# Zeros for the experts' rows in four transfers, issued with the first expert's weights behind single local tiles of the attention

## The chip, the cores and the metric

The kernel runs on one core of a Trainium2 chip. The metric is device time in microseconds (us) of one execution. All times of the profile are us from the first instruction of the span, unless ns stands beside them.

## The reference, cut to what matters

Three layers follow one another. Everything is float32.

- Attention over q, k, v of shape (2, 8, 576, 64). One part pools q, k and v by 4 along the sequence (144 positions), attends over them and repeats each result row 4 times. The other part lets each query attend to the keys fewer than 4 positions away. Their sum, 1152 tokens of 512 values, is x.
- A layer of 8 experts with top-1 routing. `w_gate` (512 x 8) gives logits, each token goes to its best expert, which takes at most 288 tokens (`capacity`), in order of the token number. An expert computes `relu(x @ w1) @ w2`, with 1024 hidden values. The result is multiplied by the token's gate probability.

```
for i in range(N):
    e = expert_idx[i]
    if counts[e] < capacity:
        disp[e, counts[e]] = x[i]
        ...
h = np.maximum(np.einsum('ecd,edf->ecf', disp, w1), 0.0)
y = np.einsum('ecf,efd->ecd', h, w2)
```

- A feed-forward layer: `h = x @ w_in` (2048 wide), `g = h * tanh(softplus(h))`, `g @ w_out`.

## The kernel before, in words

The five engines and SyncE (which issues the plain DMAs) each run a program of their own; semaphores order them. Tokens are split into 9 tiles of 128.

**Attention, 0 to about 102 us.** The work is a list `STEPS` of 15 steps: 9 local tiles ("local", t) and 6 parts of the pooled attention ("down", ...), in the order local 0 to 3, three down, local 4, three down, local 5 to 8. A loop over 19 rounds runs on TensorE, ScalarE and VectorE. In round n, TensorE computes the scores of step n (`scores`), transposes the probabilities of step n - 1 (`probs_t`) and multiplies those of an older step with v (`attend`): a down step two rounds after its scores, a local tile t in round t + 8. So local tiles 0 to 4 wait for their attend until the pooled rows are there; their probabilities, transposed, are kept in the buffer `raw` (`kept_probs`): tile t in unit `min(t, 3)`, so that tiles 3 and 4 share unit 3. `raw` has four units of 1 MB, and each later takes a quarter of an expert's weights (w1 in units 0 and 1, w2 in units 2 and 3). A unit may be loaded once the attend of the tile that it holds is done. The semaphore `s_av` counts attends, and `RANK` gives each one's place in that count.

After its attend (TensorE), tile t is copied to `x_sb` (ScalarE, `x_copy`, L686), transposed (`x_transpose`, L1302), copied (`xT`), multiplied by `w_gate` (`logits`), and VectorE computes its expert, its place and its gate (`route`, `read_counts`, `place`), and multiplies the tile by the gate (L1016, semaphore `s_gx`).

**Rows by expert.** The gated rows go to a DRAM tensor `x_by_expert` (`xe_dram` in the code), 288 rows of 512 values for each expert, and behind them 1152 rows that take the rows of dropped tokens. GpSimd scatters tile after tile with an indirect DMA (L627), after it has placed the pooled rows for all down steps (`place_od`, L592). The 2304 rows of the experts must be zero where no token lands, so SyncE first writes zeros to all of them (L472). The source is tile 8 of `x_sb`, which GpSimd has set to zero (`s_xz`) and which nobody writes until the end of the attention. The scatters, and the copy of tile 8 into `x_sb` in round 16, wait for these zeros (`s_zf`). When six scatters have landed, SyncE reads the first 256 rows of expert 0 (`load_full(0)`), and TensorE transposes them (`early_rows`); tiles 6 to 8 are added to them from `x_sb` by a matrix product with a one-hot matrix (`late_rows`), without DRAM.

**SyncE's program** up to the experts is a plain list: q and k, the pooled v, `w_gate`, the windows of v (`vwin`, L448), slot numbers (L470), then the zeros and the four units of expert 0 (L472, L477), then `load_full(0)` and the rest. Each issue runs in that order; a wait holds up all that stands behind it.

**Experts, about 114 to 263 us.** A loop over 8 experts: 64 matmuls with w1, 64 with w2, while SyncE loads the next expert's units as they become free. **Feed-forward, to the end.** Three sweeps over 384 tokens each, every product in three matmuls of float32r halves.

Of the kernel before, what the change touches and what calls it, by code (L numbers as in the profile page):

```python
# [7 lines left out]
P = 128  # L8
# [13 lines left out]
DM = H * D  # L22
E, FE = 8, 1024
# [10 lines left out]
NT = N // P  # L34
# [78 lines left out]


EARLY = 6


LAG_X = 8
HELD = NT // 2
KEPT = HELD + 1  # L120
# [6 lines left out]
def local_step(t):  # L127
    return STEPS.index(("local", t))
# [9 lines left out]
RANK = {m: i for i, m in enumerate(ATT)}  # L138
# [6 lines left out]
def build(nc, q, k, v, w_gate, w1, w2, w_in, w_out, consts, consts16, slot_nos, out, cap):  # L145
    tok_dram = nc.dram_tensor("token_of_slot", (N, 1), U32, kind="Internal").ap()
    CAP = cap

    xe_dram = nc.dram_tensor("x_by_expert", (E * CAP + N, DM), F32, kind="Internal").ap()
# [9 lines left out]
    with ctx:  # L159
        def alloc(stack, name, shape, dt, **kw):  # L160
            return stack.enter_context(nc.sbuf_tensor(name, shape, dt, **kw))

        def sem(name):
            return ctx.enter_context(nc.semaphore(name))
# [41 lines left out]
        x_sb = alloc(att, "x_sb", [P, NT, DM], F32)  # L206
# [29 lines left out]
        wo_in = alloc(exp_mem, "wo_in", [P, 2, DM], F32)  # L236
        slot_oh = alloc(exp_mem, "slot_oh", [P, NT - EARLY, SLOTS], F32)
        exp_mem.close()
# [27 lines left out]
        s_pt, s_ptc, s_av, s_avc = sem("probsT"), sem("probsT_copied"), sem("attn_out"), sem("attn_out_copied")  # L266
# [4 lines left out]
        s_xz, s_zf, s_xg, s_xet = sem("x_tile_zeroed"), sem("x_rows_zeroed"), sem("expert_x_in"), sem("expert_x_transposed")  # L271
# [63 lines left out]
        def od_copies(n):  # L335

            _, b, c, hh = STEPS[n]
            first = 0 if b == 0 else NT // 2 + 1
            cols = slice(hh * 4 * D, (hh + 1) * 4 * D)
            if c == 0:  # L340
                return [(vwin[OD_ROWS:P, 2 * (first + u):2 * (first + u) + 2, cols], slice(32 * u, 32 * u + 32)) for u in range(3)]
            out_ = []
            for half in range(2):
                cols = slice(half * 4 * D, (half + 1) * 4 * D)
                out_.append((vwin[OD_ROWS:P, 2 * (first + 3):2 * (first + 3) + 2, cols], slice(BLK * half, BLK * half + 32)))
                out_.append((vwin[OD_ROWS:P, BPB - 1 + b:BPB + b, cols], slice(BLK * half + 32, BLK * half + 64)))
            return out_
# [25 lines left out]
        def expert_units(e):  # L373

            a = w1[e].rearrange("(k p) f -> p k f", p=P)
            b = w2[e].rearrange("(k p) d -> p k d", p=P)
            return [a[:, :, 0:FE // 2], a[:, :, FE // 2:FE], b[:, 0:M1 // 2, :], b[:, M1 // 2:M1, :]]
# [43 lines left out]
        def _(sp):  # L421
# [45 lines left out]
            for g in range(BPB, NB):  # L467
# [1 line left out]

            sp.dma_start(slot_no[:, :], slot_nos).then_inc(s_sno, 16)  # L470
            sp.wait_ge(s_xz, 1)
            sp.dma_start(xe_dram[0:E * CAP, :].rearrange("(p a) d -> p a d", p=P),  # L472
                         x_sb[:, NT - 1, :].unsqueeze(1).to_broadcast([P, E * CAP // P, DM])).then_inc(s_zf, 16)

            def load_unit(e, i):

                sp.dma_start(raw[:, i, :].rearrange("p (k f) -> p k f", k=K1), expert_units(e)[i]).then_inc(s_raw[i], 16)  # L477

            for i in range(4):
                sp.wait_ge(s_av, RANK[local_step(i if i < 3 else KEPT - 1)] + 1)  # L480
                load_unit(0, i)

            def load_full(e, landed):

                sp.dma_start(xg[:, 0:XT - 1, :], xe_dram[bass.ds(e * CAP, FULL), :].rearrange("(a p) d -> p a d", p=P)
                             ).then_inc(landed, 16)
# [17 lines left out]

            sp.wait_ge(s_scat, 16 * EARLY)
            load_full(0, s_xg0)
# [52 lines left out]
        def _(pool):  # L559
# [26 lines left out]
            def place_od(n):  # L586

                pool.wait_ge(s_avc, RANK[n] + 1)
                done = od_placed(n - 1)
                for dst, rows in od_copies(n):  # L590
                    src = od[rows, n % 2, :].unsqueeze(1).to_broadcast([32, dst.shape[1], 4 * D])
                    nc.gpsimd.tensor_copy(dst, src).then_inc(s_odv, 1)  # L592
                    done += 1
                    pool.wait_ge(s_odv, done)
# [22 lines left out]
            for n in range(NS):  # L617
                if is_down(n):
                    place_od(n)
            pool.wait_ge(s_zf, 16)  # L620
            for t in range(NT):
                pool.wait_ge(s_gx, t + 1)
                if t == EARLY:
                    pool.wait_ge(s_xg0, 16)
# [56 lines left out]
        def _(act):  # L681
# [3 lines left out]
            def copy(dst, src):  # L685
                return nc.scalar.activation(dst, src, ACT.Copy)  # L686
# [35 lines left out]
            def x_copy(m):  # L722
                t = STEPS[m][1]
                act.wait_ge(s_av, RANK[m] + 1)
                if t == NT - 1:
                    act.wait_ge(s_zf, 16)
                copy(x_sb[:, t, :], ps[:, XB, :]).then_inc(s_avc, 1)

            def xt_copy(t):
# [138 lines left out]
        def _(dve):  # L868
# [14 lines left out]
            def pooled(t):  # L883


                def red(dst, src):
                    return V.tensor_reduce(dst, src.rearrange("p h (s f) -> p h s f", f=FACTOR), X, ALU.add)  # L887
                dve.wait_ge(s_qTc, t + 1)
                dve.wait_ge(s_kTc, t + 1)
                turn = ((HELD + 1) * P - S) // FACTOR  # L890
                for _, b, r0, n in tok_pieces(t):
                    lo, s0, cnt = b * S + r0, r0 // FACTOR, n // FACTOR
                    qcol = s0 if b == 0 else SDP + (s0 - turn if s0 >= turn else SD + s0)
                    kcol = b * SD + s0
                    red(qdT[:, :, qcol:qcol + cnt], qT[:, :, lo:lo + n])
                    last = red(kdT[:, :, kcol:kcol + cnt], kT[:, :, HALO + lo:HALO + lo + n])
                last.then_inc(s_qd, 1)
# [63 lines left out]
            def need(count):  # L961
                dve.wait_ge(s_r, count)
# [31 lines left out]
            def place(t):  # L994
# [10 lines left out]
                need(row)  # L1005
                if t >= EARLY:
                    if t == EARLY:
                        dve.wait_ge(s_sno, 16)
                    V.tensor_scalar(slot_oh[:, t - EARLY, :], slot_no[:, :], -float(E * CAP), r_a[:, c], ALU.add, ALU.is_equal
                                    ).then_inc(s_xoh, 1)  # L1010
# [159 lines left out]
        def _(pe):  # L1170
# [36 lines left out]
            def scores(n):  # L1207
                s0 = 2 * (n % 2)
                if STEPS[n][0] == "down":
                    _, b, c, hh = STEPS[n]  # L1210
                    for j in range(2):
                        if j == 1:
                            between(n)
                        for par in range(2):
                            for rows, q0, half in ([(slice(0, QA), 0, hh)] if c == 0 else
                                                   [(slice(BLK * i, BLK * i + BLK), QA, i) for i in range(2)]):
                                hp = 2 * half + j
                                r = slice(D * par, D * par + D)
                                q_ = qdT[r, hp, b * SDP + q0:b * SDP + (QA if c == 0 else SDP)]
                                last = mm(ps[rows, s0 + par, j * SD:(j + 1) * SD], q_, kdT[r, hp, b * SD:(b + 1) * SD], True, True)  # L1220
                else:
                    t = STEPS[n][1]
                    var = {0: 1, NT // 2: 2, NT - 1: 3}.get(t, 0)
                    for par in range(2):
                        mm(ps[:, s0 + par, 0:4 * WIN].rearrange("p (h w) -> p h w", h=4), identb[:, :],
                           maskb[:, var, :].unsqueeze(1).to_broadcast([P, 4, WIN]), True, False)
                    for hp in range(HP):
                        if hp == HP // 2:
                            between(n)
                        for j in range(2):  # L1230
                            for par in range(2):
                                r = slice(D * par, D * par + D)
                                c0 = t * P + j * BLK
                                last = mm(ps[j * BLK:(j + 1) * BLK, s0 + par, hp * WIN:(hp + 1) * WIN],
                                          qT[r, hp, c0:c0 + BLK], kT[r, hp, c0:c0 + WIN], False, True)
                last.then_inc(s_sc, 1)
# [332 lines left out]
```

## Time and profile before

| | us |
|---|---|
| three runs | 471.12, 474.72, 475.45 |
| median | 474.72 |
| the profiled execution, time | 477.65 |
| its span, first to last instruction | 475.5 |

Mean granted clock of TensorE in the profiled execution is 0.968 of 2.4 GHz. Busy shares of the span: TensorE matmul 94%, weight load 87%, VectorE 59%, ScalarE 48%, GpSimd 29%. The chain that ended last lies 84% on TensorE. In the rows further down, "issue" ahead of an instruction is idle time in which the engine waited for nothing that the profile shows; "remote" is a wait whose releaser the profile can't name. PE is TensorE's matmuls, PEld its weight loads.

### The profile page before, as it was taken

The numbers are of one execution on the slowest core, as the hardware profiler recorded it, in microseconds if no ns is written. First come the engines' busy times: TensorE is split into PE (matmuls) and PEld (weight loads), VectorE is DVE, ScalarE is ACT, GpSimd is POOL, SyncE is SP. The second block draws the span as 40 slices with busy tenths as digits, with TensorE's granted clock in tenths as the row PEclk, the third lists the DMA queues.
The fourth block names the chain that finished last, engine by engine and source line by source line (L and its number), as shares of the span: only waits on it lengthen the run. The fifth ranks groups of instructions, "written<-read, shape, count | busy, mean of one in ns | idle before, by whom it ended". The sixth has DMA issues, their size and how long they took to land.

```text
span 475.5 us, 10038 instructions
## 1 busy us (share of the span) xinstructions
PE 447.9 (94%) x3380; PEld 412.8 (87%) x3381; DVE 280.7 (59%) x665; ACT 230.1 (48%) x631; POOL 137.2 (29%) x136
## 2 busy tenths in 40 slices
PE   8869898989879999999999999999999999999993
PEld 7658687878879999999999898899988999988982
DVE  7879577679202102102111599888888888888873
ACT  2756665642313323332223566655665655656541
POOL 9587325111000000000004455433253333433202
PEclk9979899599989999999999999999999999999998
DMA  9999999232867988996846234123141121321001
GB/s 186 196 193 152 166 379 347 101 112 74 293 240 243 357 300 281 350 311 207 281 159 207 82 88 45 43 88 90 44 143 57 49 83 45 90 110 44 1 0 66
DMA packets 72143, 74.97 MB, mean 158 GB/s; under 512 B 32816, under 2 KB 47920, under 8 KB 72112
## 3 DMA queue, kind: packets, MB, share of 16 engines
q1 hardware_dynamic: 70384, 69.84, 51.0%
q0 software_dynamic: 1728, 4.72, 2.6%
q8 instruction: 18, 0.29, 0.3%
q14 instruction: 13, 0.11, 0.1%
HBM read 65.11 MB, written 9.44 MB: 157 GB/s over the span
## 4 chain that ended last, share of the span: by engine, by line
PE 84%; DVE 6%; ACT 4%; issue 3%; DMA 1%; SPq 1%; POOLq 0%; POOL 0%; ACTq 0%; DVEq 0%
PE ps L1174 79%; ACT pr L703 2%; PE ps L1256 2%; PE ps L1421 1%; DMA qk_tok<-in_q 1%; PE ps L1302 1%; SPq L431 1%; DVE mx L928 1%; DVE sme L935 1%; PE ps L1251 0%; DVE qT L901 0%; ACT prT L686 0%; DVE kdT L887 0%; DVE qdT L887 0%; DVE gL L1080 0%
## 5 line engine op out<-in xcount | busy, mean ns | idle before, releaser
L637 POOL TENSOR_TENSOR wiL<-raw,wiH 128x512 fp32r<-128x512 f32 x48 | 62.5, 1303 | 251.5 <-ACT wiH L686 148.3
L1174 PE MATMUL ps<-xe,raw 128*128 128x128 f32 (+2 forms) x512 | 71.7, 302 | 4.7 <-issue 3.9
L1174 PEld LDWEIGHTS ps<-xe,raw 128*128 128x128 f32 x512 | 70.4, 194 | 5.6 <-issue 4.4
L1174 PE MATMUL ps<-hid,raw 128*128 128x128 f32 (+2 forms) x512 | 70.8, 297 | 0.0
L1174 PEld LDWEIGHTS ps<-hid,raw 128*128 128x128 f32 x512 | 69.0, 191 | 0.0
L1174 PE MATMUL ps<-x2H,wiH 128*128 128x384 f32 x192 | 65.1, 339 | 0.3 <-DVE x2L L1080 0.3
L1174 PE MATMUL ps<-x2L,wiH 128*128 128x384 f32 x192 | 65.3, 340 | 0.0
L1174 PE MATMUL ps<-x2H,wiL 128*128 128x384 f32 x192 | 64.6, 337 | 0.0
L1174 PE MATMUL ps<-woH,gH 128*128 (+1 forms) x144 | 56.9, 395 | 2.5 <-DVE gL L1080 2.5
L1174 PE MATMUL ps<-woH,gL 128*128 (+1 forms) x144 | 57.2, 397 | 0.0
L1174 PE MATMUL ps<-woL,gH 128*128 (+1 forms) x144 | 56.7, 394 | 0.0
L1080 DVE TENSOR_TENSOR woL<-wo_in,woH 128x1024 f32 x8 | 9.8, 1226 | 79.4 <-ACT woH L686 79.4
L825 ACT ACTIVATE md<-mg 128x384 f32<-128x384 f32 x48 | 25.3, 526 | 43.8 <-DVE mg L1139 43.7
L781 ACT ACTIVATE hid<-ps 128x128 f32<-128x128 f32 (+2 forms) x64 | 18.8, 301 | 56.2 <-PE ps L1174 53.8
L1117 DVE TENSOR_SCALAR mu<-ps 128x384 f32<-128x384 f32 x48 | 26.7, 557 | 25.4 <-PE ps L1174 24.2
L1174 PEld LDWEIGHTS ps<-x2H,wiH 128*128 128x128 f32 x192 | 36.0, 188 | 2.5 <-issue 0.5
L1174 PEld LDWEIGHTS ps<-x2L,wiH 128*128 128x128 f32 x192 | 36.1, 188 | 1.9
L1080 DVE TENSOR_TENSOR x2L<-ps,x2H 128x128 f32 (+2 forms) x32 | 9.1, 321 | 46.0 <-ACT x2H L686 46.0
L1174 PEld LDWEIGHTS ps<-x2H,wiL 128*128 128x128 f32 x192 | 36.0, 188 | 0.0
L686 ACT ACTIVATE gH<-ps 128x384 fp32r<-128x384 f32 x47 | 23.2, 493 | 24.3 <-DVE ps L1151 24.3
L703 ACT ACTIVATE pr<-ps,mx 128x70 f32<-128x70 f32 (+2 forms) x96 | 30.6, 343 | 8.3 <-DVE mx L928 5.2
L1174 PEld LDWEIGHTS ps<-woH,gH 128*128 128x128 f32 x144 | 27.0, 187 | 8.0 <-DVE gL L1080 3.7
(140 smaller groups left out, 769.1 us busy)
## 6 DMA issues: line engine op xcount, KB each, us to landing
raw<-in_moe_w SPq DMA_DIRECT2D x32, 1024.0 KB
raw<-in_moe_w_in SPq DMA_DIRECT2D x24, 512.0 KB
x_by_expert<-x_sb SPq DMA_DIRECT2D x1, 4608.0 KB, 15.5
xg<-x_by_expert SPq DMA_DIRECT2D x8, 512.0 KB, 3.6
wo_in<-in_moe_w_out SPq DMA_DIRECT2D x8, 512.0 KB
v<-in_v SPq DMA_DIRECT2D x4, 576.0 KB
qk_tok<-in_k SPq DMA_DIRECT2D x8, 256.0 KB, 4.8
qk_tok<-in_q SPq DMA_DIRECT2D x8, 256.0 KB, 5.1
```

The costliest lines, as they stand in the source:

```text
L431: d = sp.dma_start(qk_tok[p0:p0 + n, slot3, i, :].rearrange("p (h d) -> p h d", h=H), src[b, :, r0:r0 + n, :].rearrange("h s d -> s h d"))
L637: nc.gpsimd.tensor_tensor(wiL[:, r, :, :], raw_wi_tile(r), wiH[:, r, :, :].bitcast(F32), ALU.subtract).then_inc(s_wil, 1)
L686: return nc.scalar.activation(dst, src, ACT.Copy)
L703: last = nc.scalar.activation(pr[0:rows, n % 2, a, h * w:(h + 1) * w], ps[0:rows, 2 * (n % 2) + a, h * w:(h + 1) * w], ACT.Exp, bias=mx[0: ...
L781: nc.scalar.activation(hid[:, m, 0:w], ps[:, m % 4, 0:w], ACT.Relu).then_inc(s_hr, 1)
L825: nc.scalar.activation(d, mg[:, r1, :], ACT.Ln, bias=2.0).then_inc(s_ln, 1)
L928: V.tensor_reduce(st(mx), sc, X, ALU.max, negate=True).then_inc(s_mx, 1)
L935: V.tensor_scalar(st(sme), st(sm), f, f * EPS, ALU.mult, ALU.add).then_inc(s_den, 1)
L1080: V.tensor_tensor(dst, whole, high.bitcast(F32), ALU.subtract).then_inc(sem_, 1)
L1117: V.tensor_scalar(mu[:, r, :], ps[:, 3 + r, 0:SW], MISH_CAP, None, ALU.min).then_inc(s_uc, 1)
L1174: return T.matmul(out_, a, b, start=start, stop=stop, skip_group_check=True)
L1256: last = T.transpose(ps[0:WIN, 6 + h // 4, (h % 4) * P:(h % 4 + 1) * P], pr[:, n % 2, h % 2, (h // 2) * WIN:(h // 2 + 1) * WIN], ident)
```

## The change

Before, the zeros are one transfer of 4608 KB, issued at once when `x_sb`'s last tile is zero, and units 0, 1, 2, 3 are issued behind the attends of local tiles 0, 1, 2 and 4. Now the zeros are four transfers of 576 rows (1152 KB) each, read from 96 instead of 128 partitions, six rows from each. The first is issued where the single one was. Then SyncE waits for the attends of local tiles 1 to 6 in turn and issues: behind tile 1 unit 0; behind tile 2 zeros 1; behind tile 3 unit 1 and zeros 2; behind tile 4 zeros 3; behind tile 5 unit 2; behind tile 6 unit 3. Both waits for the zeros want all four transfers.

```
--- before.py
+++ after.py
@@ -113,6 +113,11 @@
 
 
 EARLY = 6
+
+
+ZERO_PARTS, ZERO_P = 4, 96
+UNIT_BEHIND = {1: 0, 3: 1, 5: 2, 6: 3}
+ZERO_BEHIND = {2: 1, 3: 2, 4: 3}
 
 
 LAG_X = 8
@@ -469,16 +474,26 @@
 
             sp.dma_start(slot_no[:, :], slot_nos).then_inc(s_sno, 16)
             sp.wait_ge(s_xz, 1)
-            sp.dma_start(xe_dram[0:E * CAP, :].rearrange("(p a) d -> p a d", p=P),
-                         x_sb[:, NT - 1, :].unsqueeze(1).to_broadcast([P, E * CAP // P, DM])).then_inc(s_zf, 16)
+
+            def zero_rows(i):
+
+                rows = E * CAP // ZERO_PARTS
+                per = rows // ZERO_P
+                sp.dma_start(xe_dram[i * rows:(i + 1) * rows, :].rearrange("(p a) d -> p a d", a=per),
+                             x_sb[0:ZERO_P, NT - 1, :].unsqueeze(1).to_broadcast([ZERO_P, per, DM])).then_inc(s_zf, 16)
+
+            zero_rows(0)
 
             def load_unit(e, i):
 
                 sp.dma_start(raw[:, i, :].rearrange("p (k f) -> p k f", k=K1), expert_units(e)[i]).then_inc(s_raw[i], 16)
 
-            for i in range(4):
-                sp.wait_ge(s_av, RANK[local_step(i if i < 3 else KEPT - 1)] + 1)
-                load_unit(0, i)
+            for t in range(1, 7):
+                sp.wait_ge(s_av, RANK[local_step(t)] + 1)
+                if t in UNIT_BEHIND:
+                    load_unit(0, UNIT_BEHIND[t])
+                if t in ZERO_BEHIND:
+                    zero_rows(ZERO_BEHIND[t])
 
             def load_full(e, landed):
 
@@ -617,7 +632,7 @@
             for n in range(NS):
                 if is_down(n):
                     place_od(n)
-            pool.wait_ge(s_zf, 16)
+            pool.wait_ge(s_zf, 16 * ZERO_PARTS)
             for t in range(NT):
                 pool.wait_ge(s_gx, t + 1)
                 if t == EARLY:
@@ -723,7 +738,7 @@
                 t = STEPS[m][1]
                 act.wait_ge(s_av, RANK[m] + 1)
                 if t == NT - 1:
-                    act.wait_ge(s_zf, 16)
+                    act.wait_ge(s_zf, 16 * ZERO_PARTS)
                 copy(x_sb[:, t, :], ps[:, XB, :]).then_inc(s_avc, 1)
 
             def xt_copy(t):
```

## Rows read from the trace of the kernel before

**Rows 1.** Windows by stage: span, busy time of each engine, granted clock, DMA share, GB/s.

```profile
58.00:80.00 22.00, 21.32 (x384) 18.36 (x383) 17.10 (x78) 14.81 (x58) 6.95 (x11) 1.00 1.01 365
80.00:102.00 22.00, 20.01 (x231) 17.26 (x231) 13.28 (x71) 12.11 (x47) 4.90 (x6) 0.69 0.32 118
...
114.00:250.00 136.00, 132.02 (x983) 131.26 (x983) 22.62 (x37) 40.62 (x122) 0.03 (x1) 0.99 0.78 268
```

**Rows 2.** Timeline of SyncE: start, length, DMA issues.

```profile
56.10 0.62 SPq L472 DMA_DIRECT2D x_by_expert<-x_sb  x1
...
...
78.26 0.37 SPq L477 DMA_DIRECT2D raw<-in_moe_w  x1
```

**Rows 3.** DMA view: queue for instructions; transfers with count, size, us to landing.

```profile
q8 instruction: 18, 0.29, 0.3%
...
x_by_expert<-x_sb SPq DMA_DIRECT2D x1, 4608.0 KB, 15.5
```

**Rows 4.** Timeline of TensorE from 70 to 114 us.

```profile
71.03 1.15 PE L1174 MATMUL ps<-vwin,raw 128*64 128x64 f32 x32
...
77.07 1.15 PE L1174 MATMUL ps<-vwin,raw 128*64 128x64 f32 x32
...
80.02 0.69 PE L1174 MATMUL ps<-vwin,prT 128*64 128x64 f32 x16
80.93 0.38 PE L1174 MATMUL ps<-vwin,prT 128*64 128x64 f32 x5 [0.22 <-issue]
...
83.16 1.86 PE L1174 MATMUL ps<-wg,xT 128*128 128x8 f32 x8 [0.40 <-issue]
84.87 1.90 PE L1256 MATMUL ps<-cst,pr 128*70 128x128 f32 x8
...
89.70 1.98 PE L1174 MATMUL ps<-vwin,prT 128*64 128x64 f32 x32
...
96.35 1.35 PE L1174 MATMUL ps<-vwin,prT 128*64 128x64 f32 x32 [0.23 <-ACT prT L686]
97.63 1.06 PE L1174 MATMUL ps<-wg,xT 128*128 128x8 f32 x8
...
99.42 0.60 PE L1302 MATMUL ps<-cst,x_sb 128*128 128x128 f32 x4
...
100.69 1.15 PE L1174 MATMUL ps<-vwin,prT 128*64 128x64 f32 x32
...
105.42 2.03 PE L1174 MATMUL ps<-cst,xg 128*128 128x128 f32 x16
...
107.41 5.55 PE L1174 MATMUL ps<-slot_oh,x_sb 128*128 128x256 f32 x24
113.80 7.41 PE L1174 MATMUL ps<-xe,raw 128*128 128x128 f32 x64 [0.84 <-ACT xe L686]
```

**Rows 5.** Shorter windows around the stall, columns as in the first group.

```profile
66.00:68.00 2.00, 1.32 (x38) 1.08 (x39) 1.33 (x7) 0.25 (x1) 0.51 (x2) 1.00 1.04 395
...
80.00:83.20 3.20, 1.90 (x34) 1.44 (x33) 0.98 (x5) 0.75 (x3) 2.02 (x3) 0.99 0.99 350
83.20:96.80 13.60, 13.38 (x118) 11.56 (x120) 8.51 (x43) 8.98 (x40) 1.92 (x2) 0.50 0.23 88
```

**Rows 6.** Timeline of ScalarE and VectorE at the stall.

```profile
82.45 0.60 ACT L686 ACTIVATE xT<-ps 128x512 f32<-128x512 f32 x1 [3.59 <-remote]
...
81.72 0.17 DVE L991 TENSOR_TENSOR prod<-ps,oh 128x8 f32<-128x8 f32 x1 [2.02 <-remote]
```

**Rows 7.** Timeline of GpSimd: the scatters of gated rows.

```profile
78.94 1.15 POOL L627 DMA_INDIRECT x_by_expert<-x_sb,xslot  x1 [0.29 <-POOL vwin L592]
...
81.66 0.96 POOL L627 DMA_INDIRECT x_by_expert<-x_sb,xslot  x1 [0.31 <-issue]
...
98.52 0.96 POOL L627 DMA_INDIRECT x_by_expert<-x_sb,xslot  x1 [5.42 <-DVE x_sb L1016]
```

## The prediction

> **What bounds the kernel now.** I read the windows by stage first. TensorE is busy 21.32 of 22 us from 58 to 80, and 132.02 of 136 us in the experts [rows 1]: there it is the bound at full clock, and the change, all of whose instructions lie between 56 and about 92 us, can only touch these later stages through a load that comes too late. From 80 to 102 it is busy 20.01 of 22 us as well, but with a granted clock of 0.69 [rows 1]. That is the weak place, and the shorter windows show it in two parts. From 80.0 to 83.2 TensorE works only 1.90 of 3.20 us at full clock. From 83.2 to 96.8 it is busy 13.38 of 13.60 us at 0.50, so at 1.2 GHz instead of 2.4 [rows 5]. The timeline says the same in instructions: the attend of local tile 5 begins at 80.02, breaks off into groups with idle time put down to "issue", and the logits behind it begin only at 83.16 [rows 4]; an undisturbed attend takes 1.15 us [rows 4]. So the stall costs 3.14 - 1.15 = 2.0 us, and the slow stretch follows directly on it. VectorE and ScalarE slept through the same time, 2.02 and 3.59 us, for releasers the profile calls remote [rows 6], although TensorE had issued its scores and transposes before 80.02. It is therefore no shortage of work, but something that held up several engines at once. What ran beside it: the DMA engines at 350 GB/s [rows 5], the load of unit 3, issued at 78.26 [rows 2], and three scatters back to back, 78.94 to 82.62 [rows 7].
>
> **The four zero transfers.** The single one took 15.5 us to land for 4608 KB [rows 3]. At the 365 GB/s of that stage [rows 1], 4.72 MB take 12.9 us, so 2.6 us are start and completion. A quarter (1.18 MB) moves in 3.2 us and a unit (1.05 MB) in 2.9 us. The added issues cost SyncE about 0.62 us each, as the one at 56.10 did [rows 2], three times 0.62 = 1.9 us, and nobody waits for SyncE there. Before, SyncE itself hung on full queues: the issue of unit 1 at 62.66 took 3.63 us where one into an idle queue takes 0.37 [rows 2]. That goes away; it gains nothing, since SyncE has slack. Reading from 96 partitions instead of 128 is not shown in the trace; the bounds are nothing and, if the engines that read were fewer by a quarter, 3.2 / 3 = 1.1 us more for each transfer, 4.3 us in all. I take nothing, since 576 rows still make 36 for each of 16 DMA engines.
>
> **When the zeros are there now.** Before at 56.10 + 15.5 = 71.6. Now zeros 2 goes behind unit 1 at the end of tile 3's attend, 71.03 + 1.15 = 72.2 [rows 4]; both move 2.23 MB in 6.1 us, with the 2.6 us they land at 80.9. Zeros 3, issued at 77.07 + 1.15 = 78.2, lands 3.2 us behind, at 84.1. GpSimd's first scatter, at 78.94 before [rows 7], then waits until 84.1, and tiles 0 to 4 follow at the pace of rows 7, (81.66 - 78.94) / 2 = 1.36 us: all five are issued by 84.1 + 6.8 = 90.9. Who waits for that: scatter 5, which its tile's gate releases at 98.52 [rows 7], about 92.5 if the stall and the slow clock are gone. Slack remains, 1.6 to 7.6 us. Behind scatter 5 stand `load_full(0)` and TensorE's transposes of its rows at 105.42 [rows 4]. So the later zeros cost nothing as long as they land before about 85.7; 4.3 us more (the 96 partitions) would eat the small slack and cost up to 2.7 us. ScalarE's wait for the zeros, before the copy of tile 8, comes at about 101.8 and is long over.
>
> The Trainium skill, "DMA: Bandwidth & Descriptors", section "Anatomy of one DMA — SWDGE (gpsimd) path", speaks against splitting: every DMA has about 2.0 us that don't shrink with size, most of it the receipt of the last write, longest when it goes to HBM. By it as an estimate three more transfers in a chain would land 6 us later, at 90, and delay the experts' rows by about 4 us. The trace has 2.6 us for the same thing, but here each transfer is queued behind the one before it and they overlap; only the last one's counts, which the sum above has.
>
> **The four units.** Unit 0 is read first at 113.80 [rows 4], and w2's units about 7.4 us later. Units 2 and 3 now go behind the attends of tiles 5 and 6. With the old timing these end at about 82.5 and 89.70 + 1.98 = 91.7 [rows 4], so unit 3 lands by 91.7 + 2.9 + 2.6 = 97.2. The cover is 113.80 + 7.4 - 97.2 = 24 us; these moves cost nothing. Nothing stands behind the waits in SyncE's list that is due before scatter 5 has landed (101 us).
>
> **What may be gained.** Only the stall and what follows it. In the stretch from tile 5's attend to tile 7's (80.02 to 96.35, 16.33 us) lie two rounds [rows 4]. A round with scores at full clock, from rows: attend, scores and transposes from 77.07 to 80.02 are 2.95 us, logits and probabilities from 97.63 to 99.42 are 1.79 us: 4.74 us, without any wait between. With waits: tile 3 to tile 4 took 77.07 - 71.03 = 6.04 us with a pooled attend of about 0.9 us in it: 5.1 us. I take 5.15 a round, as these rounds depend on ScalarE in the same way. So 16.33 - 10.3 = 6.0 us to be gained; bounds 16.33 - 2 x 4.74 = 6.85, and below nothing, since the change may make the stall longer (below). A smaller one: from 66 to 68 TensorE is busy 1.32 of 2 us with the queues at 395 GB/s [rows 5], 0.68 us, gone if full queues are its cause.
>
> **The sum** is made against the profiled execution, 477.65 us (span 475.5 and 2.15 around it). If the stall goes: 477.65 - 6.0 = 471.65. The profiled execution is 2.9 us above the median of the three runs, and one of those three, 471.12, lies where a run without the stall would: I read the three as a sign that the stall does not come in each run. The changed kernel's forecast is then 471.7, 3.0 us (0.6%) below the median.
>
> **Rivals.**
>
> - *The stall only moves (0.33; 474.7 us).* For it: the DMA engines are just as full from 72 to 87 us as before, by the sum above, and the scatters are still back to back, now beside units 2 and 3. Against it: before 80 us the engines ran 22 us beside 365 GB/s without a stall like that [rows 1]. The time is then that of the runs of before.
> - *Code fetch (0.13; 473.2 us).* The groups of TensorE's instructions with "issue" before them look like code that comes too slowly, behind megabytes of weights; the profile has 18 transfers for instructions on a queue of their own, 0.3% of the DMA engines [rows 3]. Then fewer pending transfers make the stall shorter, not absent: I give it half of what the forecast gains on the median, 474.7 - 1.5 = 473.2. The skill's "Runtime: NRT & Kernel Launch", "Instruction fetch mechanics", has each sequencer refill itself by its own DMA queue and says this is mostly hidden. Against this rival is that two other engines, which were only waiting for a semaphore, slept too [rows 6].
> - *The burst gets longer (0.12; 480.7 us).* This is the one on the slow side. If scatters issued back to back beside weight loads are what holds up the engines, the change makes it worse: five in a row from 84.1 to 90.9, beside units 2 and 3, instead of three beside one unit. The stall grows by 2.2 us (two more scatters at rows 7's pace, less their gaps) and the slow clock begins some 8 us later, so that it covers the transposes at 105.42 and the one-hot products at 107.41, 2.03 + 5.55 = 7.6 us of pure TensorE work [rows 4], of which half, 3.8 us, is lost. That is +6.0 on the median. It decides from the point where the slow stretch, 13.6 us long before [rows 5], starts after about 92.
> - *The change does nothing it says (0 apart from the first rival):* the semaphores fix the order, so the transfers must move.
>
> **How the numbers follow.** Forecast 0.42, rivals 0.33, 0.13 and 0.12. The likeliest is 471.7. A difference under 1% (4.7 us, so 470.0 to 479.5) is about what a measurement of this kernel can tell from none. Faster than 470.0 needs the forecast plus the 0.68 us and a round at its bound, 471.65 - 0.68 - 0.85 = 470.1, and a little luck: two fifths of 0.42 give 0.17, with the rest 0.18. Slower is the last rival, 0.12. All else is 0.70. The range: from 470.1 less 0.9 for the spread of runs, 469.2, to 478.3, which has the moved stall in a run like the profiled one; left out are the slow rival and a small lower tail.
>
> **What the profile after should show.** The scatters start at about 84 instead of 78.94; zeros in four transfers; VectorE and ScalarE without a remote wait of more than 1 us between 80 and 83; the clock row without halves between 82 and 97; tile 7's attend at about 90.3. If the clock row shows a half stretch beginning anywhere from 84 to 92, the stall has moved, and tile 8's attend tells the price. I am wrong in the mechanism if the stall comes at 80 to 83 although no scatter runs there; in the slack if scatter 5 follows scatter 4 without idle time; and in the size if the stall is an effect of that one profiled execution and the runs never had it.

## The result: 0.7% slower, and the profile after

The changed kernel takes 477.01 us (median of 20 runs, 472.87 to 482.45), the kernel before 474.29 us (20 runs, 471.12 to 482.49). The ratio is 1.0068, with a 95% interval of 1.0044 to 1.0091. The forecast was 471.7 us, 0.6% the other way. The profiled execution of the changed kernel took 477.73 us, its span is 475.6; that of the one before was 475.5. The two spans are equal, so the traces show where time moved, and only the timed runs show that the change loses. All ratios here and below leave out the executions more than 1.5% above the fastest of the same kernel (3 and 2 of these 20, but 5 of 12 in f1 and 6 of 12 in f2, against none of 6 in e1, f4 and f5), and the means of all executions give 1.0050 here, 1.0106 for e1, 1.0029 for f1, 1.0089 for f2, 1.0104 for f4 and 1.0077 for h2.

The windows by stage of the changed kernel (columns as in [rows 1]):

```profile
58.00:80.00 22.00, 21.66 (x362) 18.86 (x361) 16.32 (x77) 14.86 (x58) 5.86 (x10) 0.92 0.72 222
80.00:102.00 22.00, 18.39 (x272) 15.44 (x263) 14.96 (x79) 12.40 (x48) 6.18 (x6) 0.84 0.78 280
...
114.00:250.00 136.00, 132.13 (x982) 131.37 (x983) 22.86 (x37) 40.47 (x122) 0.28 (x1) 0.99 0.79 268
```

From 58 to 80 us the DMA engines now move 222 GB/s instead of 365, from 80 to 102 they move 280 instead of 118 [rows 1]: the transfers have moved backwards, as meant. TensorE is busy 18.39 of 22 us in the second stretch, less than the 20.01 before, at a clock of 0.84 instead of 0.69. The experts from 114 us on are the same.

SyncE's issues of the changed kernel show the four zero transfers (one at 55.88, one at 65.63, two merged in the piece from 73.82 on) and, at 98.83, the load of expert 0's rows:

```profile
55.88 0.66 SPq L482 DMA_DIRECT2D x_by_expert<-x_sb  x1
...
65.63 0.61 SPq L482 DMA_DIRECT2D x_by_expert<-x_sb  x1
...
73.82 6.20 SPq L482 DMA_DIRECT2D x_by_expert<-x_sb  x2
...
98.83 0.37 SPq L500 DMA_DIRECT2D xg<-x_by_expert  x1
```

GpSimd's scatters, to be held beside [rows 7]:

```profile
87.76 1.15 POOL L642 DMA_INDIRECT x_by_expert<-x_sb,xslot  x1 [7.92 <-issue]
89.22 0.96 POOL L642 DMA_INDIRECT x_by_expert<-x_sb,xslot  x1 [0.30 <-issue]
...
93.24 0.96 POOL L642 DMA_INDIRECT x_by_expert<-x_sb,xslot  x1 [0.30 <-issue]
94.51 0.96 POOL L642 DMA_INDIRECT x_by_expert<-x_sb,xslot  x1 [0.30 <-issue]
```

The first starts at 87.76 instead of 78.94, for the last zeros landed at 86.87. Six follow one another, each 0.30 us behind the last: scatter 5, at 94.51, has no wait for its tile's gate before it any more, as the one at 98.52 had before. This is what the prediction had named as the sign that its slack was not there. VectorE had multiplied that tile by its gate 1.9 us earlier:

```profile
92.15 0.49 DVE L1031 TENSOR_SCALAR x_sb<-x_sb,r_gate 128x512 f32<-128x512 f32 x1
```

Still, the sixth scatter goes out 4.0 us earlier than in the profile of before (98.52), which had its stall ahead of it.

TensorE, to be held beside [rows 4]:

```profile
81.21 1.15 PE L1189 MATMUL ps<-vwin,prT 128*64 128x64 f32 x32
...
86.07 1.15 PE L1189 MATMUL ps<-vwin,prT 128*64 128x64 f32 x32
...
90.74 1.15 PE L1189 MATMUL ps<-vwin,prT 128*64 128x64 f32 x32 [0.19 <-ACT prT L701]
...
93.58 0.17 PE L1189 MATMUL ps<-wg,xT 128*128 128x8 f32 x1 [0.26 <-issue]
...
95.01 1.23 PE L1271 MATMUL ps<-cst,pr 128*70 128x128 f32 x5 [0.61 <-issue]
...
98.40 1.98 PE L1189 MATMUL ps<-vwin,prT 128*64 128x64 f32 x32
...
104.14 3.56 PE L1189 MATMUL ps<-cst,xg 128*128 128x128 f32 x16
...
114.20 4.06 PE L1189 MATMUL ps<-xe,raw 128*128 128x128 f32 x34 [0.99 <-ACT xe L701]
```

The attends of tiles 5 and 6 at 81.21 and 86.07 and that of tile 7 at 90.74 run at full clock: the stall at 80 to 83 is gone. But there is another one, from 92.6 to 96.6: the logits break off in pieces at 93.58, and VectorE and ScalarE sleep through it for remote releasers, 4.07 and 5.34 us against 2.02 and 3.59 [rows 6]:

```profile
96.71 0.17 DVE L991 COPY lg<-ps 128x8 f32<-128x8 f32 x1 [4.07 <-remote]
...
96.61 0.60 ACT L701 ACTIVATE x_sb<-ps 128x512 f32<-128x512 f32 x1 [5.34 <-remote]
```

Tile 8's attend comes at 98.40 instead of 100.69, the transposes of expert 0's rows at 104.14 instead of 105.42, and, as their clock falls once more (3.56 us for what took 2.03 [rows 4]), the experts at 114.20 instead of 113.80. All that was won up to tile 7's attend is gone there. The rows of expert 0 had landed at 102.44, and TensorE's transposes of them show no wait for them: in this execution the stall and the clock hold up TensorE, and not the zeros. The same kernel's second profile, f4 below, says the same.

### The profile page after: what moved, and what is told of

Its sections match the earlier page's. It is cut to its first block, busy times and chain, and to the rows that moved or that the text cites. A ratio compares the mean times of both kernels' runs of the same rounds, so it can differ in the third digit from the quotient of the medians.

```text
span 475.6 us, 10041 instructions
## 1 busy us (share of the span) xinstructions
PE 445.9 (94%) x3380; PEld 410.9 (86%) x3381; DVE 280.4 (59%) x665; ACT 229.4 (48%) x631; POOL 137.3 (29%) x136
## 4 chain that ended last, share of the span: by engine, by line
PE 77%; DVE 7%; ACT 5%; DMA 4%; issue 3%; another core or an unknown queue 1%; SPq 1%; POOL 0%; POOLq 0%; DVEq 0%; ACTq 0%
PE ps L1189 73%; ACT pr L718 3%; DMA xg<-x_by_expert 2%; PE ps L1436 1%; PE ps L1317 1%; DMA qk_tok<-in_q 1%; DMA x_by_expert<-x_sb,xslot 1%; DVE sme L950 1%; SPq L436 1%; DVE mx L943 1%; PE ps L1266 1%; DVE sme L939 0%; DVE qT L916 0%; DVE kdT L902 0%
```

## The experiments

Ratios are to the kernel before, on the same chip in the same hour, with a 95% interval; four such groups were measured (the kernels whose names begin with e, f, g and h), each on another chip. "Rows in" below is the time when the load of expert 0's rows had landed.

**Is it the zeros or the units?** Four kernels take the change apart. The first two:

```
e1_zeros_only:  UNIT_BEHIND = {0: 0, 1: 1, 2: 2, 4: 3}     # zeros as changed, units as before;
                                                           # SyncE's loop over tiles 0 to 4
e2_units_only:  one zero transfer as before, and
-    sp.wait_ge(s_av, RANK[local_step(i if i < 3 else KEPT - 1)] + 1)
+    sp.wait_ge(s_av, RANK[local_step((1, 3, 5, 6)[i])] + 1)
```

Expected of the first: 

> The zeros in four transfers as in the changed kernel, the units behind local tiles 0, 1, 2 and 4 as before. Theory A (scatters issued back to back beside weight loads hold up all engines, and a longer burst holds them longer): the zeros still land after the gates of tiles 0 to 2, at about 84 to 87 us, so the burst has 4 or 5 scatters; but the units are all loaded by then, so there is little load beside the burst: the stall is shorter than the 4 us of the changed kernel, the time at or below the kernel before (ratio 0.990 to 1.003). Theory B (the length of the burst alone decides): stall of 3 to 4 us as in the changed kernel, ratio 1.004 to 1.010. Theory C (the moved units do the harm): ratio within 0.3% of 1.

Expected of the second: 

> The zeros in one transfer as before, the four units behind local tiles 1, 3, 5 and 6 as in the changed kernel. The scatters begin at about 79 us as before, three in a row, but units 0 and 1 are then done and unit 2 starts only at about 81 to 82. Theory A: the burst runs beside idle queues or the first part of unit 2, the stall at 80 to 83 is gone or under 1 us, ratio 0.988 to 0.997. Theory B: the stall of 2 us stays, ratio within 0.3% of 1. Theory C (the moved units do the harm): ratio 1.004 to 1.010.

Measured: e1 1.0125 (1.0078 to 1.0173), e2 0.998 (0.9946 to 1.0013). The delayed zeros alone lose as much as the whole change; the moved units alone lose nothing. And e1 loses although its profile has no stall of all engines at all. Its scatters (first and sixth), the load behind them, and TensorE:

```profile
88.69 1.15 POOL L642 DMA_INDIRECT x_by_expert<-x_sb,xslot  x1 [10.99 <-issue]
...
95.44 0.96 POOL L642 DMA_INDIRECT x_by_expert<-x_sb,xslot  x1 [0.30 <-issue]
...
98.16 0.37 SPq L500 DMA_DIRECT2D xg<-x_by_expert  x1
...
101.81 3.78 PE L1189 MATMUL ps<-cst,xg 128*128 128x128 f32 x16 [2.90 <-DMA xg<-x_by_expert]
...
112.10 6.07 PE L1189 MATMUL ps<-xe,raw 128*128 128x128 f32 x52 [1.00 <-ACT xe L701]
```

Here the chain can be read off without disturbance: last zeros in at 87.8, first scatter 88.69, sixth 95.44, the load issued when that has landed, 98.16, and TensorE waits 2.90 us for "DMA xg" until 101.81. Before that it had nothing else to do, and its clock was at the lower level, 1.2 GHz, from 95.2 to 105.5. None of the theories had this: A wanted at most 1.003, B a stall of 3 to 4 us, C no difference. Beside g3 below, a profile of the kernel before that is nearly undisturbed, the experts start 4.3 us later (112.10 against 107.84), 0.9% of the time. That is what late zeros cost without a stall, as an estimate from two profiles. The execution with this profile, 473.41 us, is the fastest of e1's six (median 477.08), so whether the others have a stall is not known.

**Is it the split or the delay?**

```
f1_split_upfront:  UNIT_BEHIND as in e1, ZERO_BEHIND = {}
-    zero_rows(0)
+    for i in range(ZERO_PARTS):
+        zero_rows(i)
```

> The zeros in four transfers of 96 partitions, but all four issued at once where the single one was; the units behind local tiles 0, 1, 2 and 4 as before. This is the split without the delay. Theory Z (what costs is that the last zeros land at 87 to 88 us, because six scatters at 1.27 us each, the landing of the sixth, and the load of expert 0's rows follow one another behind it, until TensorE's transposes at about 101.8): the zeros land at 71 to 73, ratio within 0.3% of 1. Theory S (splitting or the 96 partitions cost by themselves): zeros land 4 us later or more, ratio above 1.004.

Measured 0.9971 (0.992 to 1.0022). The kernel loses nothing that can be measured if the four are issued at once. But the transfers are slower, which was not expected: the first is issued at 57.00 and the last lands at 77.03, so they took 20.0 us where the single one took 15.5, with the DMA engines full in both (311 GB/s from 58 to 76 us, against 377 from 58 to 71). Here this costs nothing, for the first scatter starts only at 79.19. Between f1 and e1 lies one thing only, when zeros 1 to 3 are issued, and their intervals do not touch (they ran on two chips); neither do those of f1 and of f4 and f5 below, all three on one chip.

**How does it grow with the delay?** Zeros 1 to 3 one tile earlier (f2), as in the changed kernel (f4), and zeros 2 and 3 one tile later (f5):

```
f2_zeros_one_tile_earlier:  ZERO_BEHIND = {1: 1, 2: 2, 3: 3}
f4_changed_again:           ZERO_BEHIND = {2: 1, 3: 2, 4: 3}
f5_zeros_one_tile_later:    ZERO_BEHIND = {2: 1, 4: 2, 5: 3}
```

> The changed kernel with zeros 1, 2 and 3 behind local tiles 1, 2 and 3 instead of 2, 3 and 4. Theory Z: the last zeros land at about 80 to 81, the first scatter follows at about 81, six times 1.27 us later is 88.7, before the gate of tile 5 at about 91, so the chain no longer starts at the zeros; TensorE's transposes of expert 0's rows at about 98 to 99 where nothing else disturbs; ratio 0.996 to 1.002. Theory S or C (split or moved units): ratio 1.004 to 1.010 as for the changed kernel.

> The changed kernel itself, beside the three others on one chip, for a second profile. Theory Z: the stall of all engines at 92.6 to 96.6 us of its first profile comes or not, but TensorE's transposes of expert 0's rows start no earlier than about 101 in either case, with a wait on the load of these rows if there is no stall; ratio 1.005 to 1.012. If the stall were the cause, a profile without it would show the experts at 107 to 108 us instead of 112 to 114.

> The changed kernel with zeros 2 and 3 behind local tiles 4 and 5 instead of 3 and 4. Theory Z: the last zeros land some 3 us later than in the changed kernel, at about 90, and all behind them is later by as much: transposes of expert 0's rows at about 104.5, ratio to before about 0.006 above the changed kernel's, 1.012 to 1.018. Theories in which the zeros' landing is not the start of the chain: the same ratio as the changed kernel.

Measured: f2 1.0047 (0.999 to 1.0105), f4 1.0124 (1.0068 to 1.0181), f5 1.0127 (1.0078 to 1.0177). The intervals of f2 and f4 overlap, and so do the means of all their executions (1.0089 and 1.0104): that less delay loses less is not shown. f2's middle value lies outside theory Z's 0.996 to 1.002 and within what it gave to the split or the moved units. Its last zeros landed at 83.04, and its sixth scatter (97.25) waits 3.98 us for its gate: if f2 loses at all, its profile doesn't show late zeros as the reason. And more delay did not lose more, where 0.6% were expected. f5's profile has the later chain, even 3 us later than foreseen (last zeros in at 93.57 instead of about 90; scatters one and six, then TensorE):

```profile
94.46 1.15 POOL L642 DMA_INDIRECT x_by_expert<-x_sb,xslot  x1 [15.36 <-issue]
...
100.97 0.96 POOL L642 DMA_INDIRECT x_by_expert<-x_sb,xslot  x1 [0.30 <-issue]
...
107.36 3.66 PE L1189 MATMUL ps<-cst,xg 128*128 128x128 f32 x16 [3.15 <-DMA xg<-x_by_expert]
...
117.53 0.71 PE L1189 MATMUL ps<-xe,raw 128*128 128x128 f32 x4 [0.99 <-ACT xe L701]
```

In f4's profile the last zeros landed at 83.43, and the stall held up tile 5's gate for longer than that, so its sixth scatter waits for the gate, as before:

```profile
94.85 0.96 POOL L642 DMA_INDIRECT x_by_expert<-x_sb,xslot  x1 [4.33 <-DVE x_sb L1031]
```

f5's experts start 5.1 us later than f4's (112.43), and yet f5's span is only 2.0 us longer (476.2 against 474.2). Two things give some back. Its stall, 3.4 us of ScalarE's sleep at 94.7 to 98.1, falls behind the last attend (94.15), where TensorE has to wait for the rows anyway, while f4's, 3.8 us of TensorE's idle time up to 90.4, lies ahead of tile 7's attend. And from the start of the experts to the feed-forward layer it takes 146.9 us against 150.0, for TensorE's clock did not fall after the gap in which expert 0 ends and expert 1 begins. Whether these two make up the whole 0.6% in the timed runs is not shown.

**Do the stalls matter, and what makes them?** Theory A had the scatters in a row beside a weight load as their cause. Two kernels take the burst away from the load or apart:

```
e3_one_in_flight:  in the loop of the scatters, before each
+    if 0 < t < EARLY:
+        pool.wait_ge(s_scat, 16 * t)
e4_burst_idle:
-    pool.wait_ge(s_gx, t + 1)
+    pool.wait_ge(s_gx, max(t + 1, 5))
```

> The kernel before, but each of scatters 1 to 5 waits until the one ahead of it has landed, so that two never are in flight together. Theories A and B: no stall of all engines between 79 and 90 us, no slow stretch of TensorE's clock behind it, ratio 0.985 to 0.995 (as much as 6 us of the profiled execution). Theory D (the stall comes from something else, such as code fetch, and the scatters only happen to be there): stall and time as before, ratio within 0.3% of 1. If scatter 5 is held up past 98.5 us, up to 2 us are lost again.

> The kernel before, but the first scatter waits for the gate of tile 4, so that five scatters follow one another from about 86 to 92 us, when all four units have landed and no other transfer runs. Theory A: no stall of all engines at all, ratio 0.985 to 0.995. Theory B: a stall of about 4 us as in the changed kernel, with a slow stretch behind it, ratio 1.003 to 1.010. Theory D (not the scatters): the stall stays at 80 to 83 us although no scatter is there.

Measured: e3 1.0149 (1.0098 to 1.02), e4 1.0051 (1.0013 to 1.0088). Neither profile has the stall, as theory A expected, and yet both kernels are slower, where it expected them to be faster. In e3 the attend of tile 8 is at 93.5, 7 us earlier than in [rows 4], but a scatter goes out 3.5 us or more behind the one before, the sixth at 101.4, and TensorE's transposes wait 8.09 us for the rows, until 107.68. In e4 the sixth goes out at 97.0, and they wait 2.25 us, until 103.39 (this profile is of one of its slower executions, 477.98 against a median of 474.15). In both the zeros are as early as before and only the scatters are late: a late sixth scatter costs time without late zeros, and in these two profiles without a stall.

The next pair asks for the burst with no load near it, in the kernel before and in the changed one, and g3 is the kernel before itself:

```
g1_unit3_behind_tile7:         local_step(i if i < 3 else 7)
g2_changed_loads_after_burst:  UNIT_BEHIND = {1: 0, 3: 1, 7: 2, 8: 3}
```

> The kernel before with one edit: unit 3 is issued behind the attend of local tile 7 instead of tile 4, so that nothing is being loaded while scatters 0 to 3 are issued at 79 to 85 us. Theory A (scatters back to back beside a weight load hold up all engines): no stall at 80 to 83, no slow stretch behind it, the zeros as early as before, so tile 8's attend at about 93 to 95, TensorE's transposes of expert 0's rows at 97 to 100, the experts at 106 to 109; ratio 0.985 to 0.996. Theory B (the burst alone): stall as before, ratio within 0.3% of 1.

> The changed kernel with units 2 and 3 behind local tiles 7 and 8 instead of 5 and 6. The zeros are as late as in the changed kernel, but the burst of five or six scatters at 84 to 94 us has no load beside it but the first ones. Theories A and Z together: no stall of all engines, tile 8's attend at 93 to 94, but TensorE then waits for the rows of expert 0 until about 100 to 102 with its clock falling to the lower level, so little is won: ratio 1.003 to 1.012. If the stall alone made the changed kernel slower, ratio below 1.000.

> The kernel before itself, timed against itself, for what a comparison of two equal kernels shows here (a ratio within 0.5% of 1) and for a second profile. Theory A: its three scatters at about 79 to 83 us meet the load of unit 3 again, with a stall of all engines of about 2 us right after 80 and a slow stretch of TensorE's clock behind it. If the stall is a matter of one execution, it is absent here.

Measured: g1 1.0061 (1.0036 to 1.0087), g2 1.01 (1.0068 to 1.0132), g3 1.0 (0.9968 to 1.0032). g3 is the most useful, for it is a nearly undisturbed execution of the kernel before, with a gap of 1.06 us at 80 and a span of 469.7. Scatters 4 and 5, the load, TensorE:

```profile
86.72 0.96 POOL L627 DMA_INDIRECT x_by_expert<-x_sb,xslot  x1 [4.67 <-DVE x_sb L1016]
91.13 0.96 POOL L627 DMA_INDIRECT x_by_expert<-x_sb,xslot  x1 [3.45 <-DVE x_sb L1016]
...
93.85 0.37 SPq L485 DMA_DIRECT2D xg<-x_by_expert  x1
...
97.88 3.60 PE L1174 MATMUL ps<-cst,xg 128*128 128x128 f32 x16
...
107.84 3.88 PE L1174 MATMUL ps<-xe,raw 128*128 128x128 f32 x32 [0.84 <-ACT xe L686]
```

The gates of tiles 4 and 5 hold the scatters up here (4.67 us before the one at 86.72), so the sixth goes out 3.4 us earlier than in the changed kernel, the load at 93.85 instead of 98.83, and the experts start at 107.84 instead of 114.20. The rows had landed at 97.39, 0.5 us before TensorE took them up. (1.6 us of the load's 5.0 lie behind the sixth scatter: 4.3 us from it to the load in the changed kernel's profile, which issues unit 3 at 87.26, against 2.7 in g3.) The same for g1:

```profile
91.91 0.96 POOL L627 DMA_INDIRECT x_by_expert<-x_sb,xslot  x1 [3.38 <-DVE x_sb L1016]
...
90.94 0.37 SPq L477 DMA_DIRECT2D raw<-in_moe_w  x1
98.81 0.37 SPq L485 DMA_DIRECT2D xg<-x_by_expert  x1
...
102.40 3.43 PE L1174 MATMUL ps<-cst,xg 128*128 128x128 f32 x16 [3.55 <-DMA xg<-x_by_expert]
...
112.19 6.03 PE L1174 MATMUL ps<-xe,raw 128*128 128x128 f32 x48 [0.84 <-ACT xe L686]
```

Its sixth scatter goes out at 91.91, nearly as early, but unit 3 was issued 1 us ahead of it, and the load is issued only at 98.81, 6.9 us after the scatter instead of 2.7. TensorE waits 3.55 us. A weight load that is queued ahead of the sixth scatter costs 0.6%, about as much as the whole change did at first (1.0068). That was not foreseen, and it bears on g2 as well: units 2 and 3, issued at 94.40 and 98.47, stand around its sixth scatter (97.10), the load follows 5.7 us behind it, and its rows are in at 107.6. (g2's profile is of its slowest execution, 481.41 against a median of 475.64, and tile 4's attend was already 5.4 us later than in g3.)

The last three therefore issue units behind the load of expert 0's rows:

```
h1: unit 3, h3: units 2 and 3, of the kernel before; h2: units 2 and 3 of the changed kernel
(each taken out of the place where it stood)
     load_full(0, s_xg0)
+    for i in range(2, 4):       # h1: only 3
+        load_unit(0, i)
```

> The kernel before, with unit 3 issued right behind the load of expert 0's rows instead of behind local tile 4. So no weight load stands in the queues when scatters 0 to 5 go out, and none stands ahead of scatter 5 or of that load, as one did with unit 3 behind tile 7 (scatter 5 at 91.9, the load only at 98.8). Theory Z (the experts start some 10 us after expert 0's rows are in, and these wait for zeros, scatters and whatever loads are queued ahead of scatter 5): rows in at about 97, experts at 107 to 108, as in the undisturbed profile of the kernel before; with no long stall in most executions the ratio is 0.992 to 0.999. Theory N (the order of the unit loads does not matter, only the zeros' lateness does): ratio within 0.3% of 1. If the experts now wait for unit 3, ratio above 1.003.

> The changed kernel with units 2 and 3 issued right behind the load of expert 0's rows instead of behind local tiles 5 and 6. The zeros stay late, the loads no longer meet the scatters. Theory Z: last zeros at 83 to 88, six scatters, landing and load in 13 to 14 us behind it: rows in at 98 to 101, experts at 108 to 111; ratio to before 0.999 to 1.005, so that about half or more of the changed kernel's loss is gone and the rest is the zeros' lateness. If all of its loss is the zeros' lateness: ratio 1.007 to 1.013 as for the changed kernel. If all of it is the unit loads: ratio below 1.000.

> The kernel before with units 2 and 3 both issued behind the load of expert 0's rows: the zeros early in one transfer, and even less beside the scatters than with unit 3 alone moved. Theory Z: the same time as with unit 3 alone moved, or up to 0.3% less if unit 2, which lands at about 80, had still met the first scatters; ratio 0.990 to 0.999. If the experts wait for w2's first half, ratio above 1.003 with TensorE idle at about 115.

Measured: h1 1.0032 (0.9994 to 1.0069), h2 1.0054 (1.0018 to 1.009), h3 0.9989 (0.9955 to 1.0023). h2 is at the edge of what theory Z gave it (0.999 to 1.005). It still loses, so the late zeros cost something even with the units out of the way; whether moving the units gives anything back is not shown, for h2's interval overlaps that of the changed kernel's first measurement and that of f4. And in h2's profile, as in f4's, a stall holds up tile 5's gate, so that the sixth scatter (99.34) waits for it and not for the zeros. h3 has the shortest span of all profiles, 465.8, and its timed runs are those of the kernel before: no version beat it. h1 missed: it is not faster, where theory Z expected 0.992 to 0.999. Its experts start 4.9 us later than h3's (112.20 against 107.35): 1.5 us of that are there at tile 5's attend, and the profiles show a slow stretch of TensorE's clock from 85 to 95 behind its stall, which h3 does not have.

Both h2 and h3 also settle theory A. They have a long stall again, at 90.6 to 93.4 and at 78.9 to 81.1, with no weight load in flight. The window of h2's (columns as in [rows 1]):

```profile
90.60:93.40 2.80, 0.00 (x0) 0.00 (x0) 0.00 (x0) 0.03 (x1) 2.19 (x3) 1.00 0.58 224
```

For 2.8 us TensorE, VectorE and ScalarE do nothing whatever, while GpSimd issues scatters. So loads beside the burst are not needed for it, and theory A fell. Over all 16 profiles: 15 have three or more scatters in a row. In nine of these VectorE and ScalarE both wait 2 us or more for a remote releaser within that burst (before, changed, f1, f2, f4, f5, h1, h2, h3); in six no engine does (e1, e2, e4, g1, g2, g3), nor in e3, which has no burst. What decides in which execution it comes stays open. Its length may not be independent of the zeros: VectorE's wait in it is 2.02, 2.81, 2.81 and 2.78 us in the kernels whose zeros are early (before, f1, h1, h3), with three scatters in a row, and 4.07, 3.43, 4.37, 3.89 and 5.33 us in those whose zeros are late (changed, f2, f4, f5, h2), with four to six; ScalarE's shows no such difference. Six in a row without a stall (e1, e4, g2) occur as well. Shorter gaps put down to "issue" on TensorE alone are another matter: 1.06 us at 80 in g1 and g3, and 2.34 us at 66 to 68 in g2, before any scatter.

## Why the prediction was wrong, point by point

**The step that failed** is "When the zeros are there now ... Slack remains, 1.6 to 7.6 us". Its parts:

- The last zeros landed at 86.87, where 84.1 was worked out (83.4 in f4; 87.8 in e1, where unit 3 is issued right ahead of them). In the changed kernel's profile 1.2 us of that come from tile 3's attend, which ended at 73.4 instead of 72.2, and 1.6 from the transfers: 13.5 us from the pair's issue to the last landing instead of 11.9.
- The prediction put the cost of four transfers from 96 partitions at nothing, with a bound of 4.3 us. f1 has 4.5 us more than the single transfer (20.0 against 15.5), so the bound was nearer. No run separates the 96 partitions from the splitting.
- The pace of 1.36 us a scatter was right: (94.51 - 87.76) / 5 = 1.35. The 0.9 us from the last landing to the first scatter were left out.
- So the slack was not there. Tile 5's gate was ready at 92.64, and the sixth scatter could have gone out 0.28 us later, as in g3, at 92.9 (the guess was 92.5). It went out at 94.51: 1.6 us late, where 1.6 to 7.6 us of slack were forecast. In e1 it is 4.6 us late (95.44 instead of 90.8). The upper end, 7.6, came from an execution whose stall had held up the gate until 98.52. "The later zeros cost nothing as long as they land before about 85.7" had the right form; the limit was about 85.3 in the changed kernel's profile and 83 in e1's.
- Behind the sixth scatter lie its landing and the row load, in e1 98.16 - 95.44 = 2.7 and 101.81 - 98.16 = 3.65 us, and then nothing else for TensorE to do. The prediction had seen that these stand there and gave them no price, since it took the attention's rounds for the critical path. In g3, which has no long stall, the rows are in only 0.5 us before TensorE takes them up; it is in the stalled executions that TensorE comes later than the rows, by 1.7 us in the changed kernel's profile, 2.7 in f4 and 3.3 in h2.

So two things are shown: delaying the zeros makes the kernel slower (e1 and f4 against f1), and a late sixth scatter does so too, with the zeros as early as before (e3, e4). How the 0.7% divides between this chain and the stall in the executions that have one is open, for both profiles of the changed kernel are of the stalled kind.

**The gain** was sized rightly for its stretch: from tile 5's attend to tile 7's the changed kernel's profile takes 90.74 - 81.21 = 9.5 us instead of 16.3, 6.8 us less, where 6.0 were forecast with a bound of 6.85, and tile 7's attend comes at 90.74 where 90.3 was named. But from there to tile 8's attend it takes 7.66 us (4.15 in e1), in a new stall. And it is not the change's to give: g3, the kernel before, has tile 8's attend at 93.1 instead of 100.69 and a span 5.8 us shorter. The three runs of before had been read rightly as "the stall does not come in each run", and then 471.65 was still set as the time of the changed kernel against a median that already held such runs.

**The stall.** The changed kernel lost the one at 80 to 83, as forecast, and got one of 4.0 us at 92.6, as the rivals "the stall only moves" and "the burst gets longer" said. The latter's size, 2.2 us more, fits that one profile (4.0 against 2.0), and VectorE's waits in the other profiles point the same way. But weight loads beside the burst, the rival's condition, are not needed for a stall (h2, h3), and e1, e3 and e4 are slower although their profiles have none. So the rival had the right sign, its time, 480.7, was too high, and whether longer stalls are a part of the loss is neither shown nor excluded. Code fetch is neither shown nor excluded: TensorE's groups with "issue" look alike in all stalls.

**What held.** Splitting costs the kernel nothing as long as nobody waits for the later landing (f1, 0.9971). The Trainium skill's "DMA: Bandwidth & Descriptors", "Anatomy of one DMA — SWDGE (gpsimd) path", has some 2.0 us of fixed cost for each DMA on the path of GpSimd's transfers; the zeros are issued by SyncE. By the estimate that the prediction worked out from it, three more transfers would land 6 us later, where the prediction held that only the last one's cost counts; f1's four took 4.5 us longer than the one. Whether that is this cost or the 96 partitions is open. The single DMAs of the chain show such a cost too: 2.7 us from the issue of the sixth scatter to that of the load which waits for it, and 3.65 us from there to TensorE for 512 KB. Moving the units alone costs nothing (e2, 0.998); the cover of 24 us was ample.

## What to carry to other kernels

A transfer that looks early by 20 us (the zeros had landed at 71.6, the sixth scatter went out at 91.1 in g3 and at 98.5 in the profile of before) can be the head of a chain: follow every wait behind it to the engine that bounds the kernel, and add up each issue, landing and load on the way. Measure the slack in an execution without disturbance, as one that is stalled anyway lends it to everything: here it was 0.5 us in g3's profile. When DMAs are spread out, look at what is queued ahead of the few small ones that someone waits for: a 1 MB load issued 1 us ahead of one of these cost 4 us in g1's profile (6.9 us instead of 2.7).

## What was not expected of the hardware

- While GpSimd issues indirect DMAs in a row, one each 1.27 us, VectorE and ScalarE can wait 2.0 to 5.3 us for releasers that the profile can't name, and TensorE stands still or moves in small groups; seen in nine of 15 profiles with such a burst, in h2 also with no other transfer in flight. The cause is open.
- The same kernel, profiled twice, had spans of 475.5 and 469.7 us; the experts start at 113.80 and 107.84. Of these 6.0 us 1.8 are there at tile 5's attend (80.02 and 78.19), and the rest lies behind it, where the first has the stall and TensorE's clock at the lower level from 83.2 to 96.8, the second a gap of 1.06 us and the lower level from 97.8 to 101.2.
- From the first expert's start to the feed-forward layer the kernels took 146.7 to 147.9 us when TensorE's clock stayed at 2.4 GHz after the gap between experts 0 and 1, and 149.4 to 150.8 us when it fell for 3.4 to 6.9 us: 2 to 3 us that are won or lost there, whatever was changed ahead of it.
